# Seven block products for eight in the up projection of experts two to four

## The reference

```python
for e in range(E):                       # E = 4, w1[e]: 512 x 1024, w2[e]: 1024 x 512
    h = np.maximum(x @ w1[e], 0.0)
    out += p[:, e:e + 1] * (h @ w2[e])
...
h = x @ w_in                             # 512 x 2048
g = h * np.cos(h)
return g @ w_out                         # 2048 x 512
```

## Time and profile before

| what | us or share |
|---|---|
| median of 3 runs | 654.84 (654.76 to 655.35) |
| the profiled execution | 654.78 |
| its span, first to last instruction | 653.0 |
| PE busy | 642.1, 98% |
| DVE, ACT, POOL busy | 259.6, 235.7, 163.6 |
| mean granted TensorE clock | 1.000 |

### The profile page before, as it was taken

The page is one execution under the profiler, slowest core; times in us unless marked ns, Lnnn a source line. Parts: engine busy times, 40 slices in busy tenths (PEclk is TensorE's granted clock), DMA queues, the critical chain, the costliest instruction groups (busy, mean ns, idle before and its releaser), DMA issues.

```text
span 653.0 us, 10127 instructions
## 1 busy us (share of the span) xinstructions
PE 642.1 (98%) x3728; PEld 576.5 (88%) x3728; DVE 259.6 (40%) x638; ACT 235.7 (36%) x514; POOL 163.6 (25%) x222
## 2 busy tenths in 40 slices
PE   7899999999999999999999999999999999999998
PEld 5787889999999999999999999998999999999996
DVE  6755321212121212121212122316766576767664
ACT  6676311232111133111133111137554567644552
POOL 6683200154000154000055000068300049500000
PEclk9999999999999999999999999999999999999999
DMA  9865100033000044000034000023200003001011
GB/s 288 258 196 150 68 0 1 6 126 127 1 1 0 1 129 128 0 0 0 0 100 153 6 0 1 1 66 106 86 1 1 1 33 97 2 0 48 0 49 48
DMA packets 21892, 37.21 MB, mean 57 GB/s; under 512 B 2784, under 2 KB 14048, under 8 KB 21856
## 3 DMA queue, kind: packets, MB, share of 16 engines
q1 hardware_dynamic: 20688, 36.71, 17.7%
q10 hardware_dynamic: 1168, 0.02, 0.1%
HBM read 34.36 MB, written 2.36 MB: 56 GB/s over the span
## 4 chain that ended last, share of the span: by engine, by line
PE 96%; DVE 2%; issue 1%; ACT 1%; DMA 1%; POOL 0%; SPq 0%; DVEq 0%
PE bank L865 46%; PE bank L892 45%; PE bank L857 2%; PE bank L821 1%; PE bank L841 1%; DVE arena L613 1%; PE bank L911 1%; DMA arena<-in_k 1%; ACT arena L440 0%; DVE arena L690 0%; DVE arena L628 0%; ACT x_hi L453 0%; POOL arena L387 0%; DVE arena L633 0%; SPq L248 0%
## 5 line engine op out<-in xcount | busy, mean ns | idle before, releaser
L361 POOL TENSOR_TENSOR w_lo<-w_raw,w_hi 128x128 fp32r<-128x128 f32 (+2 forms) x180 | 138.1, 798 | 370.5 <-ACT w_hi L471 368.4
L865 PE MATMUL bank<-x_hi,w_hi 128*128 128x384 f32 (+1 forms) x576 | 196.9, 342 | 0.0
L865 PE MATMUL bank<-x_hi,w_lo 128*128 128x384 f32 (+1 forms) x576 | 194.7, 338 | 0.0
L865 PE MATMUL bank<-x_lo,w_hi 128*128 128x384 f32 (+1 forms) x576 | 193.5, 336 | 0.0
L892 PE MATMUL bank<-w_hi,hp_hi 128*128 128x512 f32 x432 | 170.9, 396 | 0.1
L892 PE MATMUL bank<-w_hi,hp_lo 128*128 128x512 f32 x432 | 170.3, 394 | 0.0
L892 PE MATMUL bank<-w_lo,hp_hi 128*128 128x512 f32 x432 | 168.1, 389 | 0.0
L647 DVE SCALAR_TENSOR_TENSOR hp_lo<-bank,hp_hi 128x384 fp32r<-128x384 f32 x96 | 53.3, 557 | 264.4 <-ACT hp_hi L476 264.4
L476 ACT ACTIVATE hp_hi<-bank 128x384 fp32r<-128x384 f32 x96 | 46.9, 491 | 278.1 <-PE bank L865 275.8
L865 PEld LDWEIGHTS bank<-x_hi,w_hi 128*128 128x128 f32 x576 | 108.3, 188 | 7.1 <-issue 1.0
L865 PEld LDWEIGHTS bank<-x_lo,w_hi 128*128 128x128 f32 x576 | 108.3, 188 | 4.9
(11 more groups left out here) (55 smaller groups left out, 346.2 us busy)
## 6 DMA issues: line engine op xcount, KB each, us to landing
w_raw<-in_weights SPq DMA_DIRECT2D x43, 512.0 KB, 3.6
arena<-in_q SPq DMA_DIRECT2D x12, 192.0 KB, 4.8
result<-arena SPq DMA_DIRECT2D x9, 256.0 KB, 2.1
w_raw<-in_weights SPq DMA_DIRECT2D x8, 256.0 KB, 6.3
arena<-in_k SPq DMA_DIRECT2D x8, 224.0 KB, 5.9
arena<-in_v SPq DMA_DIRECT2D x4, 384.0 KB, 5.1
arena<-in_v SPq DMA_DIRECT2D x4, 320.0 KB, 8.1
arena<-in_k SPq DMA_DIRECT2D x4, 192.0 KB, 3.6
```

What stands on the lines that cost most here:

```text
L361: last = nc.gpsimd.tensor_tensor(w_lo[:, f, at:at + part], raw[:, at - begin:at - begin + part], w_hi[:, f, at:at + part], ALU.subtract)
L865: last = nc.tensor.matmul(ps[:, 0:TOK], w[:, f, chunk(c)], x[:, c, token_cols(t)], start=c == 0 and i == 0, stop=c == DC - 1 and i == 2)
```

## The change

For experts two to four, tiles 0 and 1 and two hidden chunks are handled together (a group; four groups an expert, `GROUPS`). The up projection of such a group is a 2 by 2 by 2 product of blocks: two hidden chunks, two halves of the 512 input features, two tiles. It was 8 block products of 6 matmuls each (48); now it is the 7 products of Winograd's form of Strassen's scheme (42). The third tile is computed as before (`pe_alone`), and so are the first expert and the cosine blocks.

For that, sums of the weights (S1 to S4, `sum_weights`) and of the inputs (T1 to T4, `t_sum`) are formed by POOL, split into parts by ACT (`high_sums`, `t_high`) and POOL (`low_sums`, `t_low`), and DVE adds the products in `h_raw` (one copy of the first by ACT, `keep_first`; seven adds a group). The group's four hidden cells are then split (`pair_high`, `pair_low`, both from `h_raw`).

Up products, in pairs and in the third tile, now use two banks (0 and 1) in turn; the outputs of tile 0 are added up in banks 2, 3 and 7, those of tile 1 in 4, 5 and 6. PE's order in a group is: four products, two output products (of the group before; in the first group those of the third tile of the expert before), three products, two output products. Low parts of weights are made by POOL in parts of 256 columns for these experts. `ex_lo` (the sums' low part) frees a slot of `w_raw`. Between experts and cosine, three cosine `up`s are interleaved with the last two expert `down`s. The shared arena in SBUF becomes separate tensors.

```diff
-            with sp.Fori(1, BLOCKS) as e:
+            with sp.Fori(1, E) as e:
                 for f in range(FC):
-                    sp.wait_ge(w_lo_done, e * FC + f - STAGE + 1)
...
+                    sp.wait_ge(ex_lo_done, e * FC + (f - STAGE + 1))
+                    load_block(e, f)
...
+            def t_sum(n, a, b, op):
...
+                nc.gpsimd.tensor_tensor(t_now, a, b, op).then_inc(t_summed, 1)
...
+            def sum_weights(e, g):
...
+                pool.wait_ge(w_lo_done, e * FC + f + 2)
+                nc.gpsimd.tensor_tensor(a22, a21, a22, ALU.add).then_inc(s_summed, 1)
+                nc.gpsimd.tensor_tensor(a21, a11, a21, ALU.subtract).then_inc(s_summed, 1)
+                pool.wait_ge(s_summed, n + 2)
+                nc.gpsimd.tensor_tensor(a11, a22, a11, ALU.subtract).then_inc(s_summed, 1)
+                pool.wait_ge(s_summed, n + 3)
+                nc.gpsimd.tensor_tensor(a12, a12, a11, ALU.subtract).then_inc(s_summed, 1)
...
             with pool.Fori(1, E) as e:
-                for f in range(FC):
-                    low_weights(f, e * FC + f, 2 * DM)
+                low_weights(0, e * FC, PART)
+                low_weights(1, e * FC + 1, PART)
+                sum_weights(e, 0)
+                low_weights(2, e * FC + 2, PART)
+                low_sums(e, 0)
+                low_weights(3, e * FC + 3, PART)
+                sum_weights(e, 1)
+                low_sums(e, 1)
+                for g in (2, 3):
+                    low_weights(2 * g, e * FC + 2 * g, PART)
+                    low_weights(2 * g + 1, e * FC + 2 * g + 1, PART)
+                    sum_weights(e, g)
+                    low_sums(e, g)
...
+            def act_pairs(e):
+
+                for g in range(GROUPS):
+                    keep_first(e, g)
+                    pair_high(e, g, 0)
+                    if g + 1 < GROUPS:
+                        high_sums(e, g + 1)
+                    pair_high(e, g, 1)
+                    pair_high(e, g, 2)
+                    if g < 2:
+                        high_weights(4 + 2 * g, e, alone(e - 1))
+                    pair_high(e, g, 3)
+                    if g < 2:
+                        high_weights(5 + 2 * g, e, alone(e - 1))
...
+            def pair_low(e, g, i):
+                dve.wait_ge(pair_hi_done, cell_count(e, g, i))
+                nc.vector.scalar_tensor_tensor(out=hp_lo[:, i, :], in0=h_raw[:, i, :], scalar=0.0, in1=hp_hi[:, i, :],
+                                               op0=ALU.max, op1=ALU.subtract).then_inc(pair_lo_done, 1)
...
+                def add(place, ps, other):
+                    nc.vector.tensor_tensor(h_raw[:, place, :], ps, h_raw[:, other, :], ALU.add).then_inc(pair_taken, 1)
+
+                for g in range(GROUPS):
+                    dve.wait_ge(pair_lo_done, cell_count(e, g - 1, 3))
+                    dve.wait_ge(first_kept, kept_count(e, g))
+                    add(3, product(g, 1), 0)
+                    dve.wait_ge(pair_taken, product_count(e, g, 0))
+                    add(2, product(g, 2), 3)
+                    add(0, product(g, 3), 0)
+                    pair_low(e, g, 0)
+                    take_last(g, 0)
+                    dve.wait_ge(pair_taken, product_count(e, g, 1))
+                    add(1, product(g, 4), 2)
+                    take_last(g, 1)
+                    p7 = product(g, 5)
+                    add(2, p7, 2)
+                    pair_low(e, g, 1)
+                    add(3, p7, 3)
+                    take_last(g, 2)
+                    pair_low(e, g, 2)
+                    dve.wait_ge(pair_taken, product_count(e, g, 5))
+                    add(3, product(g, 6), 3)
+                    pair_low(e, g, 3)
...
+            def pe_pairs(e):
+                for g in range(GROUPS):
...
+                    pair_product(g, 0, a11, b11)
+                    pe.wait_ge(ex_lo_done, ex_count(e, g, 0))
...
+                    pair_product(g, 1, s2, t2)
+                    pe.wait_ge(ex_lo_done, ex_count(e, g, 1))
+                    pe.wait_ge(first_kept, kept_count(e, g))
+                    pair_product(g, 2, s1, t1)
+                    pe.wait_ge(pair_taken, product_count(e, g, 0))
+                    pair_product(g, 3, a12, b21)
...
+                        pair_outputs(e, g - 1, 2)
...
+                        pair_outputs(e, g - 1, 3)
+                    pe.wait_ge(pair_taken, product_count(e, g, 1))
+                    pair_product(g, 4, s4, b22)
+                    pe.wait_ge(pair_taken, product_count(e, g, 2))
+                    pair_product(g, 5, s3, t3)
+                    pe.wait_ge(w_lo_done, e * FC + (2 * g + 2))
+                    pe.wait_ge(pair_taken, product_count(e, g, 3))
+                    pair_product(g, 6, a22, t4)
+                    pair_outputs(e, g, 0)
+                    pair_outputs(e, g, 1)
...
+            pe_pairs(E - 1)
+            pe_alone(E - 1, inputs=True)
+
+            pe.wait_ge(x2_lo_done, OC)
+            for f in range(LAG):
+                pe.wait_ge(w_lo_done, E * FC + f + 1)
+                if f < 2:
+                    pe.wait_ge(hp_lo_done, MIX * FC - 1 + f)
+                up_cells(h_ps[f], f, 0, range(DC)).then_inc(up_done, 1)
+                if f < 2:
+                    down(FC - 2 + f, MIX * FC - 2 + f, None)
             pe_turn(E, 0, MIX, inputs=True)
```

More of the change, by code:

```diff
@@ L134, in build @@
[L134 to L148, removed]
+        acc = sb("acc", [P, NTOK, DC * TOK])
@@ L152, in build @@
         pt_ps = bank[3]
+        pair_y = ((bank[2], bank[3], bank[7]), y_ps[0:OC])
         def s_banks(m):
@@ new lines, in low_sums @@
+            def low_sums(e, g):
+                for half in range(2):
+                    pool.wait_ge(ex_hi_done, ex_count(e, g, half))
+                    for at in range(0, DM, PART):
+                        cols = slice(half * DM + at, half * DM + at + PART)
+                        last = nc.gpsimd.tensor_tensor(ex_lo[:, g, cols], w_raw[:, (2 * g + half) % STAGE, at:at + PART],
+                                                       ex_hi[:, g, cols], ALU.subtract)
+                    last.then_inc(ex_lo_done, 1)
@@ new lines, in t_high, with keep_first, pair_high @@
+            def t_high(n, out):
+                act.wait_ge(t_summed, n)
+                nc.scalar.activation(out, t_now, ACT.Copy).then_inc(t_hi_done, 1)
+            def keep_first(e, g):
+                act.wait_ge(pair_up, product_count(e, g, 0))
+                act.wait_ge(pair_lo_done, cell_count(e, g - 1, 0))
+                nc.scalar.activation(h_raw[:, 0, :], bank[g * PRODUCTS % 2][:, 0:TOK], ACT.Copy).then_inc(first_kept, 1)
+            def pair_high(e, g, i):
+                act.wait_ge(pair_taken, product_count(e, g, (2, 3, 4, 6)[i]))
+                if g == 0:
+                    act.wait_ge(down_done, alone(e - 1) * FC + (FC - CELLS + i + 1 + C_DOWN))
+                else:
+                    act.wait_ge(pair_down, cell_count(e, g - 1, i))
+                nc.scalar.activation(hp_hi[:, i, :], h_raw[:, i, :], ACT.Relu).then_inc(pair_hi_done, 1)
@@ new lines, in act_alone @@
+            def act_alone(e, sums):
+                for f in range(FC):
+                    alone_high(e, f)
+                    if not sums:
+                        if f >= LAG:
+                            high_weights(f - LAG, e + 1, alone(e))
+                    elif f in (3, 4, 5):
+                        high_weights(f - 3, e + 1, alone(e))
+                    elif f == 6:
+                        high_sums(e + 1, 0)
+                    elif f == 7:
+                        high_weights(3, e + 1, alone(e))
+                    if not sums and f >= 2:
+                        next_input_high(f - 2)
@@ L510, in act_turn @@
                         continue
[L512 to L518, removed]
+                    refill = (f - 1, e + 1, turn) if refills and f > 0 else None
+                    cosine(g, s, True, refill)
                     if inputs and f in TURNS:
@@ new lines, in take_shared @@
+            def take_shared(c, t, banks, first=False):
+                cell = acc[:, t:t + 1, c * DM:(c + 1) * DM]
+                if first:
+                    nc.vector.tensor_scalar_mul(cell, banks[c][:, :].unsqueeze(1),
+                                                p_now[:, t, c:c + 1]).then_inc(y_taken, 1)
+                else:
+                    nc.vector.scalar_tensor_tensor(out=cell, in0=banks[c][:, :].unsqueeze(1),
+                                                   scalar=p_now[:, t, c:c + 1], in1=cell, op0=ALU.mult,
+                                                   op1=ALU.add).then_inc(y_taken, 1)
@@ L678, in take_outputs, with dve_alone @@
+            def dve_alone(e, inputs=False):
+                for f in range(FC):
+                    hidden_low(f, alone(e) * FC + f, bank[f % 2])
+                    if f == 0:
+                        take_pair_tile(e, SECOND_TILE)
```

(40 more changed lines are left out.)

371 lines of the change are left out of this document (266 added, 105 removed).

## The result

The changed kernel takes 650.54 us (median of 4 runs, 650.18 to 651.93) against 655.0 (4 runs). The ratio is 0.9932, 95% interval 0.9916 to 0.9948: 4.5 us faster, where 10.4 had been forecast.

The account below looks back on a forecast made before the run. PE's matmul work was taken to bound the kernel, fewer matmuls shortening it one for one. 654.78 - 12.66 (removed matmuls) + 0.3 (product banks) + 1.95 (cosine hand-over) = 644.37, stated as 644.4 us; range 642.0 to 649.5.

Parts of the forecast that it names:

- the last sentence of the sum: SBUF layout: no row of the profile gives a price for it, so cost 0.
- my sign of being wrong: The prediction is wrong if PE's waits from 84 to 650 us sum to over 5 us.
- What is removed: Up projections of experts two to four: six matmuls fewer in each of 12 groups, 12.66 us off.
- The product banks: Two banks instead of four: 36 waits in the groups just covered, by 0.06 or 0.13 us; 0.3 us allowed.
- rival A: Late product banks: 0.1 to 0.2 us at each of 36 places, 3.6 to 7.2 us, total 647.7 to 651.3; chance 0.16.
- The cosine hand-over: First cosine `down`: PE arrives earlier and waits about 2.2 us for DVE's take of the last expert tile; +1.95 us.
- Rival C: Cosine hand-over free, DVE taking the outputs before PE comes: 642.1 to 642.7 us; chance 0.08.
- half clock: PE's small waits in the groups lower its clock; one group an expert at half clock gives 690 us; chance 0.02.
- Due times: POOL's doubled work before each expert's pairs arrives in time, tightest at the second expert, cover about 1 and 0.5 us; cost 0.
- rival B: Late weight path through POOL or ACT: about 4 us at the second expert, 2 at the others, 646 to 652; chance 0.09.
- D: DVE's adds wait for running POOL parts, up to 0.68 us each, 24 times: 16 us, total 660; chance 0.03.

Follow-up runs that it names:

- h1: Changed kernel with DVE's take in the second cosine chain and `p_now` moved, so `hp_hi`, `hp_lo`, `h_raw` have the addresses of the kernel before: 643.03 us.
- e2: Kernel before the change with only an unused 32-byte tensor behind `p_now`, moving the hp tiles by 32 bytes: 660.68 us.
- h2: As h1, but POOL's first input sum waits for DVE's first copy of token shares to `p_now`: 642.44 us.
- f4: As e4, with an unused 64-column DVE copy from PSUM ahead of the adds of each group's second and fifth product: 646.6 us.
- e3: Changed kernel with DVE's take of the last expert tile moved from the third cosine chain to the second: 648.2 us.
- e4: Changed kernel with both the unused 32 bytes behind `p_now` and DVE's take moved to the second cosine chain: 643.69 us.
- e1: Changed kernel with an unused 32-byte tensor behind `p_now`, putting the hp tiles on a multiple of 64 bytes: 646.6 us.

## Why the prediction was wrong

**The step that failed** is the last sentence of the sum: for the layout of SBUF "cost 0". The output matmuls were counted at the 0.229 of the earlier trace rows, as work the change leaves alone. They are, but each costs 0.0044 us more, 5.7 us together: h1, with the old addresses, has 0.2291, and e2 shows the loss with nothing else changed. No rival held it; all of mine were waits, and this one shows no wait anywhere, only a longer distance. So my sign of being wrong, waits of over 5 us, could not show it: they are 2.4. It alone carries the result out of the range: 650.54 - 5.7 = 644.8.

**What is removed.** 12.66 us, right. With the other terms put back (h2) the kernel is 655.26 - 642.44 = 12.8 us faster than the one before. The 0.3 us of the earlier trace rows has gone too, so the two make 12.96 possible.

**The product banks.** Right: no stall, 0.3 allowed. The cover worked out at 0.06 was 0.03 by f4, real but thin; rival A was one slower step away, at the price it named.

**The cosine hand-over.** Right in mechanism and place. 1.95 was allowed; e3 gives 2.3 and e4 against e1 2.9, from which the 0.3 of before is to be taken: 2.0 to 2.6. The traces give 2.06: 2.28 late and 0.08 lost behind it, less 0.21 and 0.09 before. (The prediction split that 0.3 into 0.05 and 0.27, since it set a start in the timeline against one in the chain; the sum is the same.) Rival C is refuted. That a wait of this length can be followed by half clock I had put at 0.02 and at another place. It was so in the profiled execution, and not in that of e1, whose wait was as long.

**POOL.** Due times were kept, rival B is refuted. But of the time before the pairs I had only looked for DVE operations with two SBUF inputs. The copy to `p_now` has one, and lost 0.5 us all the same. The Trainium skill, page "SBUF — State Buffer", section "SBUF: two separate sides", names operations in a two-port mode beside those with two SBUF inputs as taking the shared pair, and a running GpSimd instruction as holding them off to its end. h2 agrees: 1.61 us beside the sum in h1, 0.16 without it.

**D.** Refuted: the 84 adds took 545/557/558 ns (min, median, max), beside POOL working half of the time.

The terms as measured: 655.0 - 12.66 + 2.0 + 5.7 + 0.5 = 650.5, against 650.54. With 2.6 for the hand-over it is 651.1, so the match to a tenth is partly luck.

## What to carry to other kernels

When a change resizes or moves a tensor in SBUF, it may change the price of matmuls that it doesn't touch. Compare the distance between starts of unchanged matmuls first; if it moved everywhere, put an unused tensor of 32 bytes in and look again, at more than one size: of the five places here one was best, one near it, three bad. Take outputs off their banks in the chain before the one whose end PE needs, and let no long POOL operation run beside a small SBUF-to-SBUF copy that PE's next bank hangs on.

## What the runs showed of the hardware that was not expected

The distance between fp32r matmuls of 512 columns depends on where in SBUF the tiles lie that are loaded as their weights: 0.2290, 0.2334, 0.2301, 0.2330 and 0.2333 us at 0, 32, 64, 96 and 128 bytes past the old place, with nothing in the waits. When `hp_lo` alone was moved, the whole loss came in the distance ahead of its own matmul (0.2273 to 0.2334). Matmuls of 384 columns kept 0.175 to 0.176 in all. Which rule makes a place good, and whether it is the place against w or each tile's own, stays open: `w_hi` was moved once, and `w_lo` never against it.
